# A 47-point transform on four parts of TensorE's array, with batch 1's tiles moved into the mixing steps

## What is computed

```python
X = np.fft.rfft(x, axis=1)                       # x: 2 x 3008 x 256
Yr = Xr @ w_r - Xi @ w_i + b_r
Yi = Xr @ w_i + Xi @ w_r + b_i
Yr, Yi = soft_threshold(Yr, 0.01), soft_threshold(Yi, 0.01)
y = np.fft.irfft(Yr + 1j * Yi, n=3008, axis=1)
h = y.reshape(6016, 256) @ w_in                  # 256 x 2048
g = np.maximum(h, 0) + alpha * np.minimum(h, 0)
z = g @ w_out                                    # 2048 x 256
h = z @ w_in2
g = np.where(h >= 1, h, np.where(h <= -1, 0, (h + 1) ** 2 / 4))
return g @ w_out2
```

## Time and profile before

| what | us |
|---|---|
| median of 3 runs | 1176.13 |
| lowest and highest of the runs | 1175.85 and 1178.1 |
| the profiled execution's own time | 1175.93 |
| its span in the trace | 1173.8 |
| TensorE (PE) busy | 1167.1 (99% of the span) |
| VectorE (DVE), ScalarE (ACT), GpSimd (POOL) busy | 887.2, 852.6, 687.0 |

### The profile page before, as it was taken

How to read it: one execution, slowest core, us unless ns; L and a number is a source line. 1 busy time by engine, 2 the same in 40 slices (tenths; PEclk the granted TensorE clock), 3 DMA queues, 4 the chain that set the end, 5 groups by cost and what they waited for, 6 DMA issues and landing times.

```text
span 1173.8 us, 20998 instructions
## 1 busy us (share of the span) xinstructions
PE 1167.1 (99%) x6946; PEld 1138.4 (97%) x6946; DVE 887.2 (76%) x1678; ACT 852.6 (73%) x1880; POOL 687.0 (59%) x718
## 2 busy tenths in 40 slices
PE   9999999999999999999999999999999999999998
PEld 3899999999999999999999999999999999999998
DVE  4787777777777777777777787778778787878776
ACT  3445567777676777777677688888888787878776
POOL 1017647577565767666556566665757575756554
PEclk9999999999999999999999999999999999999999
DMA  9788411111121201202005500000000000000000
GB/s 354 228 258 267 153 55 44 52 42 54 54 70 40 68 28 41 95 27 68 19 5 177 197 19 2 27 1 28 1 28 1 27 1 27 1 27 1 14 15 27
DMA packets 41644, 77.61 MB, mean 66 GB/s; under 512 B 4672, under 2 KB 21184, under 8 KB 41536
## 3 DMA queue, kind: packets, MB, share of 16 engines
q1 hardware_dynamic: 38784, 67.82, 17.5%
q10 hardware_dynamic: 2752, 8.45, 2.0%
HBM read 45.97 MB, written 30.28 MB: 65 GB/s over the span
## 4 chain that ended last, share of the span: by engine, by line
PE 99%; DVE 0%; DMA 0%; issue 0%; SPq 0%; ACT 0%
PE bank L1272 45%; PE bank L1180 39%; PE bank L1146 6%; PE bank L1165 2%; PE bank L1120 2%; PE bank L1156 2%; PE bank L1131 2%; DMA x_sb<-x 0%; DVE g_sb L985 0%; DVE y_sum L881 0%; DVE bank L970 0%; DVE y_tile L1007 0%; ACT xc_hi L653 0%; DVE r L905 0%; DVE bank L975 0%
## 5 line engine op out<-in xcount | busy, mean ns | idle before, releaser
L519 POOL TENSOR_TENSOR g_lo<-g_sb,g_hi 128x376 fp32r<-128x376 f32 x510 | 505.4, 1002 | 362.5 <-ACT g_hi L784 361.6
L1272 PE MATMUL bank<-g_hi,w_out_hi 128*128 128x376 f32 x1024 | 342.8, 335 | 0.0
L1272 PE MATMUL bank<-g_hi,w_out_lo 128*128 128x376 f32 x1024 | 341.5, 333 | 0.0
L1180 PE MATMUL bank<-xc_hi,w_in_hi 128*128 128x376 f32 x896 | 302.5, 338 | 0.1
L1180 PE MATMUL bank<-xc_hi,w_in_lo 128*128 128x376 f32 x896 | 299.6, 334 | 0.0
L1180 PE MATMUL bank<-xc_lo,w_in_hi 128*128 128x376 f32 x896 | 299.0, 334 | 0.0
L784 ACT ACTIVATE g_hi<-g_sb 128x376 fp32r<-128x376 f32 x512 | 261.1, 510 | 45.6 <-DVE g_sb L985 28.7
L1272 PE MATMUL bank<-g_lo,w_out_hi 128*128 128x376 f32 x1024 | 259.6, 334 | 0.0
L1272 PEld LDWEIGHTS bank<-g_hi,w_out_hi 128*128 128x128 f32 x1024 | 192.2, 188 | 0.5
L1272 PEld LDWEIGHTS bank<-g_hi,w_out_lo 128*128 128x128 f32 x1024 | 192.7, 188 | 0.0
L1272 PEld LDWEIGHTS bank<-g_lo,w_out_hi 128*128 128x128 f32 x1024 | 184.2, 188 | 0.0
(11 more groups left out here) (84 smaller groups left out, 1528.8 us busy)
## 6 DMA issues: line engine op xcount, KB each, us to landing
gc<-group_consts SPq DMA_DIRECT2D x24, 256.0 KB, 4.5
zt<-slots_scratch SPq DMA_DIRECT2D x24, 256.0 KB, 4.0
inverse_scratch<-v_sb SPq DMA_DIRECT2D x24, 256.0 KB, 3.3
ut<-inverse_scratch SPq DMA_DIRECT2D x16, 384.0 KB, 5.1
slots_scratch<-a_sb ACTq DMA_DIRECT2D x15, 384.0 KB, 5.6
out<-y_tile SPq DMA_DIRECT2D x30, 188.0 KB, 1.9
x_sb<-x SPq DMA_DIRECT2D x17, 256.0 KB, 6.8
prep_raw<-wpack SPq DMA_DIRECT2D x16, 256.0 KB, 2.9
```

The costliest lines, as they stand in the source:

```text
L519: pool.tensor_tensor(g_lo[kind][:, :], g_sb[n % 3][:, :], g_hi[kind][:, :].bitcast(f32), ALU.subtract)\
L1180: done = pe.matmul(bank_of[:, 0:N], w_part[:, fp, w * P:(w + 1) * P], x_part[q % 2][:, xs, :], start=first and n == 0, stop=last_one and n ...
L1272: last = pe.matmul(acc_bank[k][c][:, 0:N], w[:, fp, upper * D + c * P:upper * D + (c + 1) * P], g_part[kind][:, :], start=first and n == 0 ...
```

## The change

The halves are no longer interleaved. Rows 0 to 63 of `x_sb` hold the even half (47 rows are data) and rows 64 to 127 the odd one, and `fwd_sb` is 128 by 64: the 47-point matrix once for each half. `real47` now issues four products of 64 rows by 64 columns of the array by 512 moving columns: half `h` goes to bank `h`, and the two halves `c` of the tile's columns go to partitions 0 to 63 and 64 to 127 of that bank. `a_sb` and its copies have 128 partitions instead of 96.

The scratch is two tensors. Part 0 has 64 of a tile's 96 rows, and the pairs 0 to 7 of the batch's 12 read it; part 1 has the other 32, for pairs 8 to 11. `store_a` stores one part of two tiles together, four transfers for each part of a batch. A `zt` load is two transfers of 64 partitions instead of one of 128.

Only batch 0's 8 tiles are processed first (`FIRST_TILES = 8`). Behind them TensorE waits for part 0's four stores and then does three products on zeros (`WAIT_PRODUCTS = 3`). Tiles 8 to 15 stand in steps 1 to 8, each between `forward(s)` and `mix(s-1)`. Batch 0's part 1 is stored at steps 2 to 5, batch 1's part 0 at steps 6, 8, 10, 12 and its part 1 at steps 14 to 17. Tile 0 is loaded whole. The mixing weights and the bias are loaded by SyncE ahead of the wait for the stores, and batch 1's tiles behind it. The diff, cut to its core:

```diff
@@ -17,21 +17,30 @@
 TILES_PER_BATCH = J // JT
 TILES = BATCH * TILES_PER_BATCH
 DC = D // P
-FIRST_TILES = TILES - 1
-LATE_TILES = {1: FIRST_TILES}
-LATE_STORES = {2 * n + 2: TILES_PER_BATCH + n for n in range(TILES_PER_BATCH)}
+
+
...
+SLOTS_47 = N1 + 1
+PLACES = tuple(range(0, QUARTER, 2)) + tuple(range(1, QUARTER, 4))
+
+
+FIRST_TILES = TILES_PER_BATCH
+LATE_TILES = {t - FIRST_TILES + 1: t for t in range(FIRST_TILES, TILES)}
+LATE_STORES = {2 + n: (2 * n, 1) for n in range(4)}
+LATE_STORES.update({6 + 2 * n: (FIRST_TILES + 2 * n, 0) for n in range(4)})
+LATE_STORES.update({14 + n: (FIRST_TILES + 2 * n, 1) for n in range(4)})
 FULL_TILES = 1
 X_SLOTS = 8
...
 
 
+SLOTS_OF_PART = (QUARTER // 2, QUARTER // 4)
 PARTS = ((0, P // 2, slice(0, P, 2)), (P // 2, ROWS_PAD, slice(1, P, 4)))
 
-LEAD = 6
-SCALAR_LOADS = tuple(range(FULL_TILES, X_SLOTS)) + tuple(range(TILES_PER_BATCH + 4, TILES))
 HALF_COLS = TILE_COLS // 2
-WARM_PRODUCTS = 1
+WARM_PRODUCTS, WAIT_PRODUCTS = 1, 3
...
+    places = np.array(PLACES)
     inv = np.zeros((ROWS_PAD, ROWS))
     for slot in range(N1):
...
             inv[2 * slot + half, half::2] = f
     n2 = np.arange(N2)
...
+
+    order = np.arange(2 * N2).reshape(2, HALVES, TILES_PER_BATCH, 2, 2).transpose(3, 0, 2, 1, 4).reshape(P)
+    fwd_g = fwd_g[:, order]
...
-    az = nc.dram_tensor("slots_scratch", [BATCH, SCRATCH_ROWS, D], f32, kind="Internal").ap()
+
+    az = [nc.dram_tensor(f"slots_scratch{part}", [BATCH, 2 * count * J, D], f32, kind="Internal").ap()
+          for part, count in enumerate(SLOTS_OF_PART)]
...
-    az_rows = az.rearrange("b (p j) d -> b p (j d)", j=J)
+    az_rows = [part.rearrange("b (p j) d -> b p (j d)", j=J) for part in az]
+    az_pairs = [part.rearrange("b (c h t p) d -> b c h p t d", c=2, t=2, p=QUARTER) for part in az]
     vz_rows = vz.rearrange("b (p j) d -> b p (j d)", j=J)
-    az_pairs = az.rearrange("b (h t p) d -> (b h) p t d", t=2, p=P)
```

```diff
+        def store_a(eng, t, part):
+
+            b, q = divmod(t, TILES_PER_BATCH)
+            eng.wait_ge(a_left, t + 2)
+            eng.wait_ge(a_right, t + 2)
+            partitions = PARTS[part][2]
+            eng.dma_start(az_rows[part][b, :, q * HALF_COLS * 2:(q + 2) * HALF_COLS * 2], a_sb[partitions, t:t + 2, :])\
+               .then_inc(a_stored[b][part], 16)
...
-                if t not in SCALAR_LOADS:
+                if t >= FIRST_TILES:
...
-                sp.dma_start(zt[p % SLOTS][:, :, :], az_pairs[p, :, :, :]).then_inc(zt_in[p % SLOTS], 16)
+                b, h = divmod(p, PAIRS // 2)
+                part = int(h >= SLOTS_OF_PART[0] // 4)
+                if h in (0, SLOTS_OF_PART[0] // 4):
+                    sp.wait_ge(a_stored[b][part], 16 * TILES_PER_BATCH // 2)
+                for c in range(2):
+                    sp.dma_start(zt[p % SLOTS][c * QUARTER:(c + 1) * QUARTER, :, :],
+                                 az_pairs[part][b, c, h - part * SLOTS_OF_PART[0] // 4, :, :, :])\
+                      .then_inc(zt_in[p % SLOTS], 16)
 
...
-            sp.dma_start(x_tile(0)[:, 0:HALF_COLS], x[0:P, 0:HALF_COLS]).then_inc(x_half_in, 16)
+            sp.dma_start(x_tile(0), x[0:P, :]).then_inc(x_in[0], 16)
             sp.dma_start(fwd_sb[:, :], fwd47).then_inc(fwd_in, 16)
-            sp.dma_start(x_tile(0)[:, HALF_COLS:], x[0:P, HALF_COLS:]).then_inc(x_in[0], 16)
-            for t in range(FULL_TILES, TILES - 2):
+            for t in range(FULL_TILES, FIRST_TILES):
                 load_x(t)
             load_matrices(0)
-            load_x(TILES - 2)
-            t = TILES_PER_BATCH - 1
-            sp.wait_ge(a_right, t + 1)
-            sp.dma_start(az_rows[0, 0:ROWS_PAD, t * TILE_COLS + HALF_COLS:(t + 1) * TILE_COLS],
-                         a_tile(t)[:, HALF_COLS:]).then_inc(a_stored[0], 16)
-            load_x(TILES - 1)
-            sp.wait_ge(a_stored[0], 16 * (TILES_PER_BATCH + 1))
+            sp.dma_start(wm_raw[:, :], wmix).then_inc(wm_in, 16)
+            sp.dma_start(bias_sb[:, :], bias).then_inc(bias_in, 16)
             load_values(0)
-            sp.dma_start(bias_sb[:, :], bias).then_inc(bias_in, 16)
+            load_x(FIRST_TILES)
+            load_x(FIRST_TILES + 1)
             for p in range(1, SLOTS):
                 load_values(p)
                 load_matrices(p)
+                load_x(FIRST_TILES + 2 * p)
+                load_x(FIRST_TILES + 2 * p + 1)
             sp.dma_start(alpha_sb[:, :], alpha).then_inc(const_in, 16)
             sp.dma_start(inv47[:, :], inv_in).then_inc(const_in, 16)
 
             for p in range(SLOTS, PAIRS):
-                if p == PAIRS // 2:
-                    sp.wait_ge(a_stored[1], 16 * TILES_PER_BATCH)
                 load_values(p)
                 load_matrices(p)
+                if p == SLOTS:
+                    load_x(TILES - 2)
+                    load_x(TILES - 1)
                 store_pair(p - SLOTS)
...
-                act.activation(a_tile(t)[:, 0:HALF_COLS], bank_a[0:ROWS_PAD, :], ACT.Copy).then_inc(a_left, 1)
...
+                act.activation(a_tile(t)[:, 0:HALF_COLS], bank_a[:, :], ACT.Copy).then_inc(a_left, 1)
...
-            for t in range(FULL_TILES, X_SLOTS):
+            for t in range(FULL_TILES, FIRST_TILES):
                 load_rows(act, t, 1)
             for t in range(FIRST_TILES):
                 copy_a(t, a_bank[(2 * t) % 4])
-                if t < TILES_PER_BATCH:
-                    store_a(t)
-                if t >= LEAD and t + LEAD in SCALAR_LOADS:
-                    load_rows(act, t + LEAD, 1)
-                if t == TILES_PER_BATCH:
-                    act.dma_start(wm_raw[:, :], wmix).then_inc(wm_in, 16)
+                if t % 2:
+                    store_a(act, t - 1, 0)
...
                 n, part = weight_job(s)
                 if part == 1:
                     if n == 0:
-                        act.wait_ge(a_stored[1], 16 * TILES_PER_BATCH)
+                        for part in range(2):
+                            act.wait_ge(a_stored[1][part], 16 * TILES_PER_BATCH // 2)
...
-                    store_a(LATE_STORES[s])
+                    store_a(act, *LATE_STORES[s])
...
-                dve.tensor_copy(a_tile(t)[:, HALF_COLS:], bank_a[0:ROWS_PAD, :]).then_inc(a_right, 1)
+                dve.tensor_copy(a_tile(t)[:, HALF_COLS:], bank_a[:, :]).then_inc(a_right, 1)
...
-                    pe.matmul(xt_bank[0][0:ROWS_PAD, :], zeros[:, 0:ROWS_PAD], zeros[:, 0:HALF_COLS],
+                    pe.matmul(xt_bank[0][:, :], zeros[:, 0:P], zeros[:, 0:HALF_COLS],
...
             def real47(t, banks):
-                for part, copied in enumerate((a_left, a_right)):
-                    if t == 0 and part == 0:
-                        pe.wait_ge(x_half_in, 16)
-                    else:
-                        pe.wait_ge(x_in[t], 16 if t < FULL_TILES else 32)
+                pe.wait_ge(x_in[t], 16 if t < FULL_TILES else 32)
+                for h, copied in enumerate((a_left, a_right)):
                     if t >= 2:
                         pe.wait_ge(copied, t - 1 if t < FIRST_TILES else t)
-                    pe.matmul(banks[part][0:ROWS_PAD, :], fwd_sb[:, :], x_tile(t)[:, part * HALF_COLS:(part + 1) * HALF_COLS],
-                              start=True, stop=True).then_inc(a_done, 1)
+                    rows = slice(QUARTER * h, QUARTER * (h + 1))
+                    for c in range(2):
+                        last = pe.matmul(banks[h][QUARTER * c:QUARTER * (c + 1), :], fwd_sb[rows, :],
+                                         x_tile(t)[rows, c * HALF_COLS:(c + 1) * HALF_COLS], start=True, stop=True)
+                    last.then_inc(a_done, 1)
...
-                    pe.wait_ge(zt_in[slot], 16 * uses + 16)
+                    pe.wait_ge(zt_in[slot], 32 * uses + 32)
...
             for t in range(FIRST_TILES):
-                real47(t, [a_bank[(2 * t + part) % 4] for part in range(2)])
+                real47(t, [a_bank[(2 * t + h) % 4] for h in range(HALVES)])
+            pe.wait_ge(a_stored[0][0], 16 * TILES_PER_BATCH // 2)
+            idle_products(WAIT_PRODUCTS)
             for s in range(STEPS):
                 forward(s)
                 if s in LATE_TILES:
```

34 lines of the change are left out of this document (11 added, 23 removed).

## The result

| us | before | changed | forecast |
|---|---|---|---|
| median of the runs (lowest to highest) | 1176.3 (1175.38 to 1178.1, 8 runs) | 1179.53 (1178.21 to 1180.48, 8 runs) | 1175.1 |
| the execution profiled: own time / span | 1175.93 / 1173.8 | 1178.21 / 1176.1 | |
| start of `forward(0)` | 31.61 | 24.28 | 24.2 |
| start of `mix(0)` | 34.38 | 26.28 | 26.3 |
| start of `mix(1)` | 36.65 | 30.68 | 29.6 |

The ratio of the times is 1.0026, 95% interval 1.0015 to 1.0037: slower by about 3 us, where no change or a small gain was forecast. The execution profiled is the fastest of the eight (the other spans are 1177.0 to 1178.4), so its trace shows 2.3 us of the loss. It is also one of two whose mean granted clock was 0.999; the other six have 0.996 to 0.998, and the kernel before has 0.999 or 1.000 in every execution whose clock is on record.

The account below looks back on a forecast made before the run. TensorE was taken to bound the kernel, nearly level with DMA from 8 to 26 us. Terms -7.4, +8.1 and -1.7 sum to -1.0 at `mix(7)`: 1175.93 becomes 1174.9, forecast as median 1175.1; range 1172.0 to 1187.5.

Parts of the forecast that it names:

- the rival of 1.72 and 2.15: Tile products: quarters don't run side by side, 1.72 us a tile in a row, 2.15 alone; 1185.3 to 1188.8; chance 0.26.
- the half at 1.29: Tile products: two of the four overlap fully, 1.29 us a tile; 1178.5, up to 1180; chance 0.12.
- The sum of bytes: Ahead of step 0: 6.33 MB moved up to part 0's stores, so they have landed at 19.5 us.
- The rival of early stores: Ahead of `forward(0)`: engines serve stores first, part 0 stored at 17.3 us; 1172.2 to 1173.6; chance 0.28.
- zeros at full rate: Ahead of `forward(0)`: zero products at 0.86 end at 22.1, hidden by `zt0`'s load, so `forward(0)` is possible at 23.5.
- zeros at the lower level: Ahead of `forward(0)`: three zero products at 1.2 GHz take up to 5.4 us and would end at 24.9.
- The change of mode: Steps with a tile: switching between quarter and full products costs 0.15 us a tile, between nothing and 0.7.
- the second issue of a pair: SyncE's queue ahead of `forward(0)`: issuing the second of `zt0`'s two transfers takes 0.45 us.
- The sum at `mix(7)`: Start of `mix(7)`: -7.4 from the start, +8.1 from eight tiles, -1.7 from tile 15, together -1.0 us.
- What follows is the same work bound by the same engine: Behind `mix(7)`: nothing changes, so all that its start moves moves the end.
- DMA share of 0.87: Steps with tiles: mixing 0.58 plus tiles 0.29 of DMA's rate, full but not over.
- a sign of being wrong: Wrong if TensorE waits over 1 us in all for `zt` or batch 1's tiles, or steps run at the lower clock.

Follow-up runs that it names:

- third trace: The changed kernel, unedited, timed and traced a third time beside the kernel before; ratio 1.0029 [1.0018, 1.0040].
- no zeros: Changed kernel without the three products on zeros ahead of `forward(0)`, the wait for the stores kept; ratio to the kernel before 1.0029.
- stores by SyncE: Changed kernel with batch 0's part 0 stored from SyncE's queue instead of ScalarE's; ratio to the kernel before 1.0026.
- part 1 early: Changed kernel with batch 1's part 1 stored at steps 7, 9, 11, 13 instead of 14 to 17; ratio to the kernel before 1.0028.
- the repeats: The changed kernel, unedited, timed twice more beside the kernel before; ratios 1.0033 and 1.0029.
- packed with 15 tiles first: Changed kernel with tiles 0 to 14 ahead of step 0, tile 15 in step 1, no products on zeros; ratio to the kernel before 0.9998.
- one `zt` load: Changed kernel with scratch rows reordered: each `zt` load one transfer of 128 partitions, each store two; ratio to the kernel before 1.0033.
- three tiles in the gap: Changed kernel with single `zt` loads, GpSimd's stores, tiles 8 to 10 ahead of `forward(0)`, four zero products, TensorE not waiting for stores; ratio to before 0.9991.

## Why the prediction was wrong

**Right.** The packing and the stretch up to the stores. The quarters run side by side (0.87 for the second tile; the rival of 1.72 and 2.15 is out, and so is the half at 1.29). The page of the Trainium skill that I set against my forecast (TensorE: Matmul & The Clock Gate, "Packing small matmuls") is borne out in its rule of packing; its rule of order, as I had extended it to the two instructions of a product, is not: 16 instructions take 1.88. The sum of bytes put the landing of the stores at 19.5; they landed at 19.86, 20.14 and 20.48. The rival of early stores, 17.3, is out with it.

**In part luck.** In the first trace `forward(0)` and `mix(0)` came within 0.1 of the forecast. The forecast was the middle between zeros at full rate, where 23.5 for `zt0` counts, and zeros at the lower level, 24.9. The zeros ran partly at each level and ended at 24.44. In the third trace they ran wholly at the lower one and ended at 26.01, past both bounds, and `mix(0)` was 1.7 late.

**Wrong, from `mix(0)` to `mix(7)`: 2.3 us.** Two steps of the prediction failed.
The change of mode was mis-sized. I took 0.15 a tile from the nearest row, the change from `forward` to `mix`, and wrote down 0.7 as the other end; it is 0.33. That makes 7 x 0.19 = 1.3 (steps of 3.51 for 3.32). That row was no change between full array and quarters at all. The Trainium skill's rule (TensorEngine Tiling, Key Properties), that a change of tiling mode drains the engine, agrees in so far as a change costs; no row shows the drain itself.
And SyncE's queue was counted for tile 8 and `zt`, but not for `gc1`, which stands behind them. The count stopped at the first load that TensorE waits for. Eight issues of 0.59 to 0.66 with 0.04 between them put `gc1`'s load at 25.12 and `forward(2)` at 29.05: 0.9 more. I had also priced the second issue of a pair at 0.45, from the one issue of 0.39 in the earlier trace rows. So the path that the sum followed, from the zeros through `forward(0)` and `mix(0)`, was not the one that ended last. That one runs from the landing of the stores through SyncE's eight issues to `gc1`. In the six traces with this queue behind the stores (the changed kernel's three, no zeros, stores by SyncE, part 1 early) `mix(1)` starts 10.8 to 11.1 behind the landing and `mix(7)` 31.9 to 32.2, whatever zeros and clock did ahead of `mix(0)`.
The sum at `mix(7)` was -1.0; these make it +1.2, and the first trace has 51.77 - 50.49 = 1.3. The 1.5 and 2.1 of the repeats are the same with a later landing.

**Wrong, behind `mix(7)`: 0.9 to 2 us.** "What follows is the same work bound by the same engine" did not hold. I had computed a DMA share of 0.87 for the steps with tiles and called it "full but not over", and looked no further than step 8. In the trace 26 to 50 has 0.89, near the 0.87, and TensorE had no wait for `zt` there; the waits came behind `mix(18)`, where single loads took long to land. The two traces of before have none. The prediction had named more than 1 us of such waits as a sign of being wrong: the first trace stays under it with 0.9, the repeats lose 2.1 and 1.6. Which part of the change brings them is open: splitting the `zt` loads alone shows 0.4 ahead of `mix(35)` and no measurable loss, one load instead of two left the wait ahead of `mix(19)`, and storing earlier did not remove them. The version with packed tiles and all of them first has them too (101.85), so they don't need the moved tiles. What the traces do show is that they vary from one execution to the next and that the loads waited for took 6 to 9 us, where the median of the changed kernel's `zt` loads is 3.6; the load is issued in time in the changed kernel's trace (110.68, right behind the `forward` that frees its buffer) and late, behind SyncE's weight loads, in three others (packed with 15 tiles first, one `zt` load, three tiles in the gap).

**What the idea could have given.** Before, TensorE and DMA were level ahead of step 0. Packing frees TensorE there, and nothing came of it (0.9998), since the tiles then wait for their data and run at the lower clock behind the waits; some 1.7 us of that might be had back, which was not tried. Moving the tiles frees DMA there, but opens a gap of 9 us on TensorE between the last tile and `forward(0)`, and each moved tile costs 1.20 in a step that has no room, for 0.97 saved. Three tiles put into the gap save 3.0 at `mix(7)`, which brings back the loss, no more.

## What to carry to other kernels

Small products packed into parts of the array give their full saving of engine time in a block of their own, if the data keep up; strewn one group at a time between full-array products, each group pays for two changes of mode, here 0.33 us on 0.87. Before work is moved out of a stretch that two engines bound equally, price it at both places with the engine that is then the bound. When a step gets more transfers, list every issue of its queue in order up to the last load that someone waits for, and price each by the range of durations in that queue, not by the shortest row. Ask of every wait which path ends last, and when an engine is left waiting, read the granted clock behind the wait before calling the stretch bound by data.
